# Feed-forward and last stage of a fused attention kernel in three 512-token blocks instead of four of 384

## The reference, cut to what matters

```python
def _moe_ref(x, U, V, w_ch1, w_ch2):
    xt = x.transpose(0, 2, 1)
    h = xt @ U @ V
    u = x + h.transpose(0, 2, 1)
    ch = np.maximum(u @ w_ch1, 0.0) @ w_ch2        # 512 -> 2048 -> 512
    return (u + ch).astype(np.float32)

def _moe2_ref(x, mu_k, mu_r, w_k, w_v, w_r):
    x_prev = np.concatenate([np.zeros((B, 1, D)), x[:, :-1, :]], axis=1)
    xk = mu_k * x + (1.0 - mu_k) * x_prev
    xr = mu_r * x + (1.0 - mu_r) * x_prev
    k = np.maximum(xk @ w_k, 0.0)                  # 512 -> 1024
    v = k * k @ w_v                                # 1024 -> 512
    r = 1.0 / (1.0 + np.exp(-(xr @ w_r)))          # 512 -> 512
    return (r * v).astype(np.float32)
```

## Time and profile before

| | us |
|---|---|
| median of 3 runs (529.55 to 531.17) | 530.61 |
| the profiled execution's own time | 531.21 |
| span of the profiled execution | 529.4 |
| TensorE busy | 517.7 |
| GpSimd busy | 251.3 |
| VectorE busy | 188.5 |
| ScalarE busy | 136.9 |

### The profile page before, as it was taken

How to read it: one execution, slowest core, us unless ns; L and a number is a source line. 1 busy time by engine, 2 the same in 40 slices (tenths; PEclk the granted TensorE clock), 3 DMA queues, 4 the chain that set the end, 5 groups by cost and what they waited for, 6 DMA issues and landing times.

```text
span 529.4 us, 11016 instructions
## 1 busy us (share of the span) xinstructions
PE 517.7 (98%) x4304; PEld 489.0 (92%) x4304; DVE 188.5 (36%) x527; ACT 136.9 (26%) x384; POOL 251.3 (47%) x263
## 2 busy tenths in 40 slices
PE   5999999999999999999999999999999999999997
PEld 4788888999999999999999999998998998998996
DVE  5777775123212222122221222211532432443223
ACT  4777774211011110111111111112321321321321
POOL 3255647191008100089600768901995996897000
PEclk9999999999999999999999999999999999999999
DMA  6867755122002200024400000000001001001001
GB/s 211 284 233 226 237 175 170 65 76 84 0 0 80 79 0 0 0 79 160 158 0 0 0 0 1 0 0 1 1 0 59 0 0 60 1 0 59 0 0 59
DMA packets 15345, 33.85 MB, mean 64 GB/s; under 512 B 1488, under 2 KB 1872, under 8 KB 15312
## 3 DMA queue, kind: packets, MB, share of 16 engines
q1 hardware_dynamic: 14736, 32.57, 18.3%
q10 hardware_dynamic: 576, 0.84, 0.5%
HBM read 30.25 MB, written 3.15 MB: 63 GB/s over the span
## 4 chain that ended last, share of the span: by engine, by line
PE 97%; DVE 1%; DMA 1%; issue 0%; POOL 0%; ACTq 0%; DVEq 0%; POOLq 0%
PE psum L555 25%; PE psum L567 25%; PE psum L611 13%; PE psum L620 12%; PE psum L635 6%; PE psum L415 5%; PE psum L427 3%; PE psum L449 3%; PE psum L441 1%; PE psum L457 1%; PE psum L466 1%; DVE probs L849 1%; PE psum L463 1%; DMA k_in<-in_k 1%; PE psum L464 1%
## 5 line engine op out<-in xcount | busy, mean ns | idle before, releaser
L964 DVE SCALAR_TENSOR_TENSOR HL<-psum,HH 128x384 fp32r<-128x384 f32 x64 | 35.7, 558 | 174.6 <-ACT HH L748 174.6
L748 ACT ACTIVATE HH<-psum 128x384 fp32r<-128x384 f32 x64 | 31.5, 492 | 233.2 <-PE psum L555 233.2
L555 PE MATMUL psum<-UH,w1h 128*128 (+1 forms) x256 | 86.3, 337 | 0.0
L567 PE MATMUL psum<-HH,w2h 128*128 128x384 f32 x256 | 86.1, 336 | 0.0
L567 PE MATMUL psum<-HL,w2h 128*128 128x384 f32 x256 | 86.1, 336 | 0.0
L555 PE MATMUL psum<-UH,w1l 128*128 (+1 forms) x256 | 86.0, 336 | 0.0
L555 PE MATMUL psum<-UL,w1h 128*128 (+1 forms) x256 | 85.9, 335 | 0.0
L567 PE MATMUL psum<-HH,w2l 128*128 128x384 f32 x256 | 85.8, 335 | 0.0
L1087 POOL TENSOR_SCALAR w1h<-raw 128x2048 fp32r<-128x2048 f32 x4 | 7.7, 1923 | 126.2 <-PE psum L567 126.2
L567 PEld LDWEIGHTS psum<-HH,w2h 128*128 128x128 f32 x256 | 48.1, 188 | 0.2 <-issue 0.2
L567 PEld LDWEIGHTS psum<-HL,w2h 128*128 128x128 f32 x256 | 48.1, 188 | 0.0
(11 more groups left out here) (118 smaller groups left out, 944.9 us busy)
## 6 DMA issues: line engine op xcount, KB each, us to landing
v_in<-in_v SPq DMA_DIRECT2D x16, 384.0 KB, 4.6
raw<-in_moe_w_ch SPq DMA_DIRECT2D x6, 1024.0 KB, 5.3
v_rest<-in_v_rest SPq DMA_DIRECT2D x8, 384.0 KB, 3.6
out<-result SPq DMA_DIRECT2D x12, 256.0 KB, 2.1
k_in<-in_k SPq DMA_DIRECT2D x7, 432.0 KB, 4.1
q_in<-in_q SPq DMA_DIRECT2D x7, 384.0 KB, 3.1
raw<-in_moe_w_ch SPq DMA_DIRECT2D x8, 256.0 KB, 4.3
raw<-in_moe_w_v SPq DMA_DIRECT2D x2, 1024.0 KB, 5.2
```

The lines of the kernel that those rows point to most:

```text
L555: mm = pe.matmul(bank[4 + f % 2][:, 0:BLK], w[:, kt, f * P:(f + 1) * P], x[:, kt, ds(blk * BLK, BLK)], start=kt == 0 and n == 0, stop=kt = ...
L567: mm = pe.matmul(bank[d][:, 0:BLK], w[:, f, d * P:(d + 1) * P], x[:, f % 2, :], start=f == 0 and n == 0, stop=f == FQ - 1 and n == 2)
L748: act.activation(HH[:, f % 2, :], bank[4 + f % 2][:, 0:BLK], ACT.Relu).then_inc(hid_high, 1)
L964: dve.scalar_tensor_tensor(out=HL[:, f % 2, :], in0=bank[4 + f % 2][:, 0:BLK], scalar=0.0, in1=HH[:, f % 2, :].bitcast(F32), op0=ALU.max, ...
```

## The change

BLK becomes 512 and NBLK 3. Block 1 holds the last 256 tokens of the first sequence and the first 256 of the second. The mixing keeps its halves of 384 (HALF). `Y` becomes one run of 1536 columns with a single zero column in front, so that the boundary columns of blocks need no copy; where a block contains the beginning of the second sequence, one column of the product with the token before is set to zero between the products and the sum. The two scratch tiles of the shift are renamed and lie elsewhere (the gate's inputs now fill the region of `raw`), and the scratch that the runtime keeps for dynamic DMA is 8192 bytes. A block has four tiles of 128 tokens, so `values` uses banks 0 to 3 and the gates share banks 4 and 5: the third and fourth gate tile wait for the sigmoid of the tile two before. `values` of the first block now waits for the last addition to `Y`, where the third gate tile did.

```diff
-    BLK = S // 2
+    HALF = S // 2
+    BLK = 512
...
-        Y = region("Y", [P, KT, NBLK, BLK + 1])
+        Y = region("Y", [P, KT, TOK + 1])
...
-        GATE_BANKS = [4, 5, 3]
+        GATE_BANKS = [4, 5]
...
                 for t in range(TPB):
-                    if GATE_BANKS[t] < KT:
-                        pe.wait_ge(acc_added, KT * (NQ * NBLK + 1))
+                    if t >= 2:
+                        pe.wait_ge(gate_set, TPB * j + TPB + t - 1)
                     for kt in range(KT):
                         for n, (x, w) in enumerate(((XRH, WRH), (XRH, WRL), (XRL, WRH))):
-                            mm = pe.matmul(bank[GATE_BANKS[t]][:, :], x[:, kt, t * P:(t + 1) * P], w[:, kt, :],
+                            mm = pe.matmul(bank[GATE_BANKS[t % 2]][:, :], x[:, kt, t * P:(t + 1) * P], w[:, kt, :],
...
                     if f == 2:
+                        pe.wait_ge(acc_added, KT * (NQ * NBLK + 1))
                         pe.wait_ge(result_done, TPB * j + TPB)
...
-            for blk in range(0, NBLK, 2):
-                pool.memset(Y[:, :, blk, 0:1], 0.0).then_inc(edge_done, 1)
+            pool.memset(Y[:, :, 0:1], 0.0).then_inc(edge_done, 1)
...
-                        pool.tensor_scalar(shift_a[:, :], yj[:, 1:BLK + 1], mu[:, m, d:d + 1], 0.0,
+                        pool.tensor_scalar(here[:, :], Y[:, d, at + 1:at + BLK + 1], mu[:, m, d:d + 1], 0.0,
                                            ALU.mult, ALU.add).then_inc(shift_step, 1)
-                        pool.tensor_scalar(shift_b[:, :], yj[:, 0:BLK], mu_rest[:, m, d:d + 1], 0.0,
+                        pool.tensor_scalar(ahead[:, :], Y[:, d, at:at + BLK], mu_rest[:, m, d:d + 1], 0.0,
                                            ALU.mult, ALU.add).then_inc(shift_step, 1)
...
+                        if at < S < at + BLK:
+                            pool.memset(ahead[:, S - at:S - at + 1], 0.0).then_inc(edge_done, 1)
+                            pool.wait_ge(edge_done, EDGES + KT * i + d + 1)
+                        pool.tensor_tensor(here[:, :], here[:, :], ahead[:, :], ALU.add).then_inc(shift_step, 1)
...
-                pool.tensor_copy(Y[:, :, blk, 0:1], Y[:, :, blk - 1, BLK:BLK + 1]).then_inc(edge_done, 1)
...
-    nc = bacc.Bacc("TRN2", target_bir_lowering=False, num_devices=1)
+    nc = bacc.Bacc("TRN2", target_bir_lowering=False, num_devices=1, dynamic_dma_scratch_size=8192)
```

More of the change, by code:

```diff
@@ L58, in block_kernel @@
     FIRST = 2 * P
-    assert D == 64 and RANK == 32 and ST == 6 and KT == 4 and NQ == 4 and FT2 == 8 and NBLK == 4
+    assert D == 64 and RANK == 32 and ST == 6 and KT == 4 and NQ == 4 and FT2 == 8 and NBLK == 3
     assert PPB == KT and UNITS == 3 and PAIRS == 8
@@ L114, in block_kernel @@
         XRL = region("XRL", [P, KT, BLK], F32R)
-        shift_a = region("shift_a", [P, BLK])
-        shift_b = region("shift_b", [P, BLK])
         region = Region(x_at)
@@ L147, in block_kernel @@
         WRL = region("WRL", [P, KT, DM], F32R)
+        here = region("here", [P, BLK])
+        ahead = region("ahead", [P, BLK])
         end = region.at
@@ L319, in u_slice, with y_slice @@
         def u_slice(p, half):
-            at = (2 * (p // PPB) + half) * BLK
-            return p % PPB, slice(at, at + BLK)
+            at = (2 * (p // PPB) + half) * HALF
+            return p % PPB, slice(at, at + HALF)
+        def y_slice(p, half):
+            kt, cols = u_slice(p, half)
+            return Y[:, kt, cols.start + 1:cols.stop + 1]
         def pair_x(p, t):
@@ L462, in mixed @@
                 to = bank[M_BANK]
[L463 to L467, removed]
+                cols = slice(half * HALF, (half + 1) * HALF)
+                pe.matmul(to[:, 0:HALF], A4[:, slot, :], VH4[:, cols], start=True, stop=False)
+                pe.matmul(to[:, 0:HALF], A4[:, slot, :], VL4[:, cols], start=False, stop=False)
+                for i in range(ST // 2):
+                    mm = pe.matmul(to[:, i * P:(i + 1) * P], x(half * ST // 2 + i), ident[:, :],
+                                   is_transpose=True, start=False, stop=i == ST // 2 - 1)
                 mm.then_inc(mix_done, 1)
@@ L680, in mixing @@
                     return
-                kt, _ = u_slice(p, 0)
                 act.wait_ge(mix_done, 2 * p + part)
-                act.activation(Y[:, kt, 2 * (p // PPB) + part - 1, 1:BLK + 1], bank[M_BANK][:, 0:BLK],
-                               ACT.Copy).then_inc(y_kept, 1)
+                act.activation(y_slice(p, part - 1), bank[M_BANK][:, 0:HALF], ACT.Copy).then_inc(y_kept, 1)
             def banded_attention():
@@ L768, in _ @@
                     act.wait_ge(result_done, TPB * j + t + 1)
-                    act.activation(gate[:, t, :], bank[GATE_BANKS[t]][:, :], ACT.Sigmoid).then_inc(gate_set, 1)
+                    act.activation(gate[:, t, :], bank[GATE_BANKS[t % 2]][:, :], ACT.Sigmoid).then_inc(gate_set, 1)
                 for f in range(FT2):
@@ L971, in add_to_y @@
                     dve.wait_ge(acc_done, KT * step + d + 1 + KT)
-                    y = Y[:, d, ds(blk, 1), 1:BLK + 1].rearrange("p a n -> p (a n)")
+                    y = Y[:, d, ds(blk * BLK + 1, BLK)]
                     dve.tensor_tensor(y, bank[d][:, 0:BLK], y, ALU.add).then_inc(acc_added, 1)
@@ L1059, in split_u @@
                 kt, cols = u_slice(p, half)
-                y = Y[:, kt, 2 * (p // PPB) + half, 1:BLK + 1]
+                y = y_slice(p, half)
                 pool.wait_ge(y_kept, 2 * p + half + 1)
@@ L1133, in _ @@
                 split_chunk(c)
-            PER = 2 * KT * 4
             def shift(j):
                 pool.wait_ge(acc_added, KT * (NBLK * (NQ - 1) + 2) + KT * j)
+                at = j * BLK
                 for i, m in enumerate((1, 0)):
@@ L1145, in shift @@
                     for d in range(KT):
-                        n = PER * j + 4 * (KT * i + d)
+                        n = 2 * KT * j + KT * i + d
                         if m == 1:
@@ L1149, in shift @@
                         else:
[L1150 to L1153, removed]
-                        pool.tensor_scalar(shift_a[:, :], yj[:, 1:BLK + 1], mu[:, m, d:d + 1], 0.0,
+                            to_h, to_l = UH[:, d, at:at + BLK], UL[:, d, at:at + BLK]
@@ L1155, in shift @@
+                        if n > 0:
+                            pool.wait_ge(low_shift, n)
+                        pool.tensor_scalar(here[:, :], Y[:, d, at + 1:at + BLK + 1], mu[:, m, d:d + 1], 0.0,
                                            ALU.mult, ALU.add).then_inc(shift_step, 1)
-                        pool.tensor_scalar(shift_b[:, :], yj[:, 0:BLK], mu_rest[:, m, d:d + 1], 0.0,
+                        pool.tensor_scalar(ahead[:, :], Y[:, d, at:at + BLK], mu_rest[:, m, d:d + 1], 0.0,
                                            ALU.mult, ALU.add).then_inc(shift_step, 1)
-                        pool.wait_ge(shift_step, n + 2)
@@ L1159, in shift @@
[L1159 to L1163, removed]
+                        pool.wait_ge(shift_step, 4 * n + 2)
@@ new lines, in shift @@
+                        if at < S < at + BLK:
+                            pool.memset(ahead[:, S - at:S - at + 1], 0.0).then_inc(edge_done, 1)
+                            pool.wait_ge(edge_done, EDGES + KT * i + d + 1)
+                        pool.tensor_tensor(here[:, :], here[:, :], ahead[:, :], ALU.add).then_inc(shift_step, 1)
+                        pool.wait_ge(shift_step, 4 * n + 3)
+                        pool.tensor_scalar(to_h, here[:, :], 1.0, 1.0, ALU.mult, ALU.mult).then_inc(shift_step, 1)
@@ L1164, in shift @@
+                        pool.wait_ge(shift_step, 4 * n + 4)
+                        pool.tensor_tensor(to_l, here[:, :], to_h.bitcast(F32), ALU.subtract).then_inc(low_shift, 1)
                     pool.wait_ge(low_shift, 2 * KT * j + KT * (i + 1))
                     pool.sem_inc((xk_done, xr_done)[m], 1)
+            EDGES = 5
             pool.wait_ge(split_w, NCH)
[L1168 to L1172, removed]
-                pool.tensor_copy(Y[:, :, blk, 0:1], Y[:, :, blk - 1, BLK:BLK + 1]).then_inc(edge_done, 1)
@@ L1174, in _ @@
-            pool.wait_ge(edge_done, 8)
-            for j in range(1, NBLK):
+            pool.wait_ge(edge_done, EDGES)
+            for j in range(NBLK):
                 shift(j)
```

## The result

The changed kernel takes 529.78 us (median of 22 runs, 528.10 to 530.66) against 531.00 for the kernel before in as many runs: ratio 0.9969, 95% interval 0.9956 to 0.9982. That is a gain of 1.6 us by the ratio and 1.2 by the medians, clear of the noise but small, where 6.7 was forecast; 529.78 lies outside the forecast range of 522.4 to 526.0. The profiled execution has a span of 527.9.

A forecast was written before the change was run, and what follows sets the result against it. TensorE, by number and length of matmuls, was taken as the bound. Feed-forward -5.4, last stage -1.4 and tail +0.1 sum to -6.7 us: 524.5 profiled, 523.9 as a median, range 522.4 to 526.0, holding 0.89.

The forecast's parts named there:

- What bounds the kernel: From 110 us on, only number and length of TensorE matmuls count; other engines count only where they would come late.
- rival 3: Block ends of the last stage: small stalls of some 0.5 us each, together 3 us, giving 527; chance 0.04.
- Price of a matmul: Feed-forward and last stage: columns at full clock plus fixed 13.3 ns, so 173.3 ns at 384 columns, 226.7 at 512.
- Feed-forward: 16 steps become 12 of 96 matmuls at 227.3 ns: 21.82 us a step, 261.8 against 267.2, -5.4 us.
- Last stage: Only the keys' matmuls fall, 384 to 288; a block takes 54.7 us, three 164.1 against 165.5: -1.4 us.
- The bounds: Matmul price at 512 columns between 226.7 ns (-8.0 us, 522.6) and 228.9 ns (-4.9 + 0.3, 526.0).
- The shift: GpSimd work costed at nothing: shift(1) takes 46 us within a 54.7 us block, 8 us to spare.
- Rival 2: TensorE waits for GpSimd's shift before keys of blocks 1 and 2; at 7.6 us a step, 536; chance 0.03.
- Rival 1: Feed-forward and keys: excess beyond columns grows with width, 232 ns a matmul, no change at 530.6; chance 0.04.
- Waits on TensorE: Gate tiles, feed-forward and block ends: waits on sigmoids, relu and low parts stay covered, costed at nothing.
- Just closed, no stall: Last slice of a block: high and low part take 2.1 us, at longest 2.7, under a values group of 2.72.
- the Trainium skill's rule: Sign against the gain: warm gap is columns over 2.4 GHz plus 2.5 ns, so 480 fewer matmuls return only 1.2 us.

## Why the prediction was wrong, step by step

- **What bounds the kernel: right.** TensorE is busy without a gap that its records show, from 90 us to its last matmul, before (433.9 us) and after (434.4 of 434.4); the one short wait is under rival 3.
- **Price of a matmul: this step failed.** "Both widths are columns at full clock plus the same fixed 13.3 ns per matmul" is true only where the operands are placed for it: in the feed-forward at distance 0 modulo 256 the runs show 173.3 at 384 columns and 226.7 at 512, and at the distance of 32 that the change gave project, 233.3. I took the 512 price from the values, whose pair had distance 0, and put it on project, whose pair would have 32. The prediction even held the sign of it: two prices for one width, 226.7 and 228.9, in one trace. I called them bounds. They were two distances, 0 and 64. That fewer matmuls give back a fixed part each was right: with 480 or 2016 bytes of padding a step takes 21.76, and the whole kernel is some 8 us under the kernel before (531.10 to 523.01, 531.18 to 522.90).
- **Feed-forward, the term that was mis-sized.** Forecast 21.82, measured 22.20. Of the 0.38, project gives 48 x (233.3 - 227.3) = 0.29 by its own distance, and hidden 48 x (229.2 - 227.3) = 0.09 by settling. Over eleven steps 4.2 us, and 0.3 in the first (24.68 for 19.23 + 5.12).
- **Last stage, placement too.** Forecast 54.7, measured 55.3, 55.1, 55.1. "Gates and values are 512 wide already and their number stays" was true and yet no reason for their price to stay: gates 11.20 for 10.99 (their distance went from 64 to 32), values 2.75 for 2.72 (distance 0, settling). Together 1.3 us to the end of the span. 4.2 + 0.3 + 1.3 less 0.6 that the attention happened to be shorter are the 5.2 between the span forecast (529.4 - 6.7) and 527.9.
- **The bounds were too narrow.** 228.9 ns was the dearest row; the change to `Y`'s size, which stood in the diff, was costed nowhere. Allowing the difference seen between equal matmuls once more, 228.9 + 2.2 = 231.1 ns, the feed-forward would have come to 1152 x 231.1 = 266.2 us, a gain of 1.0, and with the same on the last stage the range would have reached about 530. At its other end, 226.7 throughout is not -8.0 but -8.3, since the gates would fall too; the padded kernel came out at -8.3.
- **The shift: right.** GpSimd in order of time, shift(1) of the changed kernel, its first instructions and its last:

```profile
370.39 0.69 POOL L1158 TENSOR_SCALAR here<-Y,mu 128x512 f32<-128x512 f32 x1 [15.26 <-PE psum L642]
...
371.81 0.10 POOL L1164 MEMSET ahead<- 128x1 f32 x1
...
414.80 1.29 POOL L1170 TENSOR_TENSOR UL<-here,UH 128x512 fp32r<-128x512 f32 x1
```

  370.39 to 416.09 is 45.7 us, 46 were forecast, and the keys of block 1 begin at 425.52, 9.4 later. Rival 2 did not come.
- **Rival 1 was near in time and wrong in mechanism.** Its 232 ns a matmul and its 530.6 us are close to the 231.3 and 529.78 measured, by chance. The excess is neither per column nor due to activations as moving operands: with 480 bytes of padding the same loops run at 226.7.
- **Waits on TensorE, and rival 3: there, once, and small.** "Just closed, no stall" was wrong for the first block. VectorE's low part of the last slice, and TensorE's first matmul on it:

```profile
409.50 1.75 DVE L1013 TENSOR_TENSOR HL<-k_square,HH 128x512 fp32r<-128x512 f32 x1 [2.04 <-ACT HH L782]
...
411.30 0.50 PE L627 MATMUL psum<-WVH,HH 128*128 128x512 f32 x1
```

  The low part takes 1.75 us here while the shift runs, against 0.69 at its shortest, and ends at 411.25. The matmul starts 0.05 us later, so TensorE waited (0.3 us, by the trace's list of waits); 36 values take 8.36 us where the other blocks have 8.19. That is 0.17 us, once; not 0.5 in each block. Gate tiles cost nothing that shows (the first sigmoid ends at 362.46, and the third tile starts two tiles after 359.02, at 364.6), nor does the fourth store: from the start of the last matmul to the end of the span it is 3.7 us before and after.
- **Of the Trainium skill's rule** (page "TensorE: Matmul & The Clock Gate", section "Back-to-back issue gap", 215.8 ns at 512 columns, which the page gives for an isolated matmul): the best mean spacing of a group in any of the kernels here is 226.7. In the feed-forward, at equal placement, 384 matmuls fewer gave back 5.1 us, 13.3 ns each, not 2.5.

## What to carry to other kernels

When a tensor changes size, everything behind it moves; check how far apart, modulo 256 bytes, the two operands of each fp32r matmul lie, before and after, and also the operands of products that follow each other; where widths are equal, pad so that all agree. If one trace shows two prices for the same shape of matmul, find out what differs before using either as a bound. On top of this change 480 bytes of padding were worth four times the change as written (ratio 0.984 against 0.997), while in the kernel before they were worth nothing that could be measured.

## What the runs showed of the hardware that was not expected

All of this is for fp32r matmuls with 128 x 128 weights, each with its own weight load.

- Steady price. A long run of 512-column matmuls goes at 226.7 ns when moving and stationary operand begin at the same offset modulo 256 bytes, and slower when they do not: 32, 96 and 224 apart 233.3, 64 apart 229.0, 128 apart about 232.5. The absolute offset did not matter in the one run that shifted everything, and 512 bytes more or less never did. Other distances were not tried.
